# Expert 0's first steps placed behind each reading of the stop, ahead of the jump out of the tiles

## The reference

```
X = np.fft.fft(np.fft.fft(x, axis=1), axis=2).real       # x: 4 x 3072 x 256
...
k = np.maximum(xk @ w_k, 0.0); v = k * k @ w_v            # xk, xr: mixes with the row before
r = 1.0 / (1.0 + np.exp(-(xr @ w_r)))
x = (r * v).reshape(B * S, 256)                           # 12288 rows
...
expert_idx = np.argmax(x @ w_gate, axis=1)                # 8 experts
for i in range(N):
    e = expert_idx[i]
    if counts[e] < capacity:                              # capacity = 384
        disp[e, counts[e]] = x[i]
        ...
h = np.maximum(np.einsum('ecd,edf->ecf', disp, w1), 0.0)
y = np.einsum('ecf,efd->ecd', h, w2)
out[i] = gate_w[i] * y[expert_idx[i], pos[i]]             # 0 for rows that were not kept
```

## Time and profile before

| what | us |
|---|---|
| median of 3 runs | 610.83 |
| lowest and highest | 610.41, 610.84 |
| the profiled execution's own time | 610.44 |
| its span in the profile | 608.6 |
| PE busy | 597.7 (98% of the span) |
| DVE busy | 449.9 (74%) |
| ACT busy | 317.1 (52%) |
| POOL busy | 103.5 (17%) |

### The profile page before, as it was taken

One profiled execution on the slowest core, in us unless ns is written; L12 is line 12 of the kernel. 1 busy time (PEld: TensorE's weight loads), 2 busy tenths in 40 slices (PEclk: granted clock), 3 DMA queues, 4 the chain that ended last, 5 costly groups with the idle time before them and its releaser, 6 DMA issues.

```text
span 608.6 us, 10524 instructions
## 1 busy us (share of the span) xinstructions
PE 597.7 (98%) x3368; PEld 515.6 (85%) x3368; DVE 449.9 (74%) x1054; ACT 317.1 (52%) x668; POOL 103.5 (17%) x105
## 2 busy tenths in 40 slices
PE   8999999999999999999999999999999999999995
PEld 5878888888888788888888888788888999999995
DVE  4688888887777688889786767788884777766671
ACT  1774645454545564545454545564544565665550
POOL 0710302020202020202020202020207111011111
PEclk9999999999999999999999999999999999999999
DMA  8439946241510005201010100033105944455000
GB/s 309 151 86 186 394 147 205 93 139 53 184 52 23 2 10 195 94 1 43 23 37 2 34 1 3 29 118 122 30 1 174 326 129 140 144 191 189 28 26 26
DMA packets 42157, 62.99 MB, mean 103 GB/s; under 512 B 4582, under 2 KB 32055, under 8 KB 42108
## 3 DMA queue, kind: packets, MB, share of 16 engines
q1 hardware_dynamic: 38268, 55.88, 29.0%
q0 software_dynamic: 3840, 6.52, 3.0%
HBM read 39.90 MB, written 26.91 MB: 110 GB/s over the span
## 4 chain that ended last, share of the span: by engine, by line
PE 94%; DVE 1%; SPq 1%; issue 1%; DMA 1%; ACT 1%; POOL 0%; POOLq 0%; DVEq 0%; ACTq 0%
PE bank L299 77%; PE bank L1305 4%; PE bank L1252 3%; PE bank L1264 2%; PE bank L1237 2%; DMA first_partner<-in_x 1%; PE bank L1499 1%; PE bank L1337 1%; PE bank L1508 1%; DVE xt L928 0%; PE bank L1512 0%; PE bank L1509 0%; SPq L475 0%; SPq L486 0%; PE bank L1350 0%
## 5 line engine op out<-in xcount | busy, mean ns | idle before, releaser
L299 PE MATMUL bank<-k,wv 128*128 128x512 f32 x672 | 165.3, 396 | 0.0
L299 PE MATMUL bank<-xk,wk 128*128 128x512 f32 x642 | 164.1, 399 | 0.0
L299 PEld LDWEIGHTS bank<-k,wv 128*128 128x128 f32 x672 | 125.6, 188 | 28.9
L299 PEld LDWEIGHTS bank<-xk,wk 128*128 128x128 f32 x642 | 118.7, 189 | 25.7
L761 ACT ACTIVATE relu<-bank 128x512 f32<-128x512 f32 x114 | 67.9, 597 | 118.7 <-PE bank L299 110.1
L629 POOL DMA_INDIRECT dispatched<-rows,slot x56 | 59.2, 1057 | 371.2 <-DVE slot L1028 324.0
L1047 DVE TENSOR_TENSOR square<-relu 128x512 f32<-128x512 f32 x113 | 78.0, 691 | 32.9 <-ACT relu L761 23.7
L1042 DVE TENSOR_TENSOR k<-square,k 128x512 fp32r<-128x512 f32 x112 | 76.7, 685 | 2.9 <-ACT k L756 2.7
L756 ACT ACTIVATE k<-square 128x512 fp32r<-128x512 f32 x113 | 70.7, 626 | 10.7 <-DVE square L1047 10.2
L299 PE MATMUL bank<-down_w,he 128*128 128x256 f32 x576 | 71.9, 284 | 0.0
L299 PEld LDWEIGHTS bank<-down_w,he 128*128 128x128 f32 x576 | 70.4, 191 | 0.0
(11 more groups left out here) (142 smaller groups left out, 721.3 us busy)
## 6 DMA issues: line engine op xcount, KB each, us to landing
out_rows<-blank SPq DMA_DIRECT2D x16, 768.0 KB
raw_up<-in_moe_w SPq DMA_DIRECT2D x8, 1024.0 KB, 22.4
raw_down<-in_moe_w SPq DMA_DIRECT2D x8, 1024.0 KB
got<-dispatched SPq DMA_DIRECT2D x16, 409.5 KB, 3.2
x_area<-in_x SPq DMA_DIRECT2D x12, 384.0 KB
y<-in_x SPq DMA_DIRECT2D x9, 384.0 KB
dispatched<-blank SPq DMA_DIRECT2D x1, 3276.0 KB, 21.4
first_partner<-in_x SPq DMA_DIRECT2D x3, 384.0 KB
```

Of the source, the lines that this page charges most:

```text
L299: done = nc.tensor.matmul(bank, w, x, start=first and i == 0, stop=last and i == len(terms) - 1)
```

## The change

`walk` gets a fifth function, `leave`. Behind the reading of the stop, the case "full" now comes first: it holds `leave()` and then a jump to behind the tiles. The case "not full" stands behind that jump (`Else`), so an engine that goes on takes a branch over `leave`.

```
-    def walk(eng, before, after, last):
+    def walk(eng, before, after, last, leave):
...
                 eng.load(stop, full[0:1, n + 1:n + 2])
-                with eng.If_eq(stop, 0):
+                with eng.If_ne(stop, 0):
+                    leave()
+                with eng.Else():
                     rest(n)
...
                 last()
+                leave()
...
-                walk(sp, before, after, last)
-
-                sp.sem_inc(rows_in[0], 16)
+                walk(sp, before, after, last, lambda: sp.sem_inc(rows_in[0], 16))
...
-                walk(pool, before, lambda n: None, lambda: route(NTILE - 1))
+                walk(pool, before, lambda n: None, lambda: route(NTILE - 1), lambda: pool.sem_inc(waits_held, 1))
...
-                walk(act, before, after, lambda: route(NTILE - 1))
-                nc.scalar.activation(warm[:, 2:3], warm[:, 1:2], ACT.Copy).then_inc(act_left, 1)
+                def turned(e, i):
+                    for h in range(DH):
+                        act.wait_ge(te_full, e * DH + h + 1)
+                        nc.scalar.activation(xe[:, i, 0, h, :], tbe[h][:, 0:cap], ACT.Copy).then_inc(xe_high, 1)
+
+                def leave():
+                    nc.scalar.activation(warm[:, 2:3], warm[:, 1:2], ACT.Copy).then_inc(act_left, 1)
+                    turned(0, 0)
+                    nc.scalar.activation(warm[:, 0:1], warm[:, 1:2], ACT.Exp)
+
+                walk(act, before, after, lambda: route(NTILE - 1), leave)
...
-                turned(0, 0)
                 act.wait_ge(dve_left, 1)
...
-                walk(dve, before, after, last)
-                nc.vector.memset(least[:, :], 0.0).then_inc(dve_left, 1)
...
+                def leave():
+                    nc.vector.memset(least[:, :], 0.0).then_inc(dve_left, 1)
+                    turned(0, 0)
+
+                walk(dve, before, after, last, leave)
 
                 dve.sem_inc(he_ready, 3)
                 dve.sem_inc(ye_ready, SP)
...
                 dve.sem_inc(we_ready, PIECES)
-                turned(0, 0)
                 dve.wait_ge(act_left, 1)
...
                         up(n, 2)
                         up(n, 3)
+
+                def after(n):
+                    seq, stage = n // TILES + 1, stage_of(n)
                     if n % TILES:
                         up(n, 2)
-
-                def after(n):
-                    seq, stage = n // TILES + 1, stage_of(n)
...
-                walk(pe, before, after, last)
-
...
+                def leave():
+                    turn(0, 0, 0)
+                    pe.wait_ge(act_left, 1)
+                    keep_warm_with(5, ident, ident, hbe[1])
+
+                walk(pe, before, after, last, leave)
...
-                turn(0, 0, 0)
-                pe.wait_ge(act_left, 1)
-                keep_warm_with(3, ident, ident, hbe[1])
-                pe.wait_ge(dve_left, 1)
                 with pe.Fori(0, EXPERTS // 2) as turn_no:
```

More of the change, by code:

```diff
@@ L1164, in last, with turned @@
                     dve.wait_ge(routed, NTILE + 2)
-                walk(dve, before, after, last)
-                nc.vector.memset(least[:, :], 0.0).then_inc(dve_left, 1)
+                def turned(e, i):
+                    for h in range(DH):
+                        dve.wait_ge(xe_high, e * DH + h + 1)
+                        nc.vector.tensor_tensor(xe[:, i, 1, h, :], tbe[h][:, 0:cap], xe[:, i, 0, h, :].bitcast(fp32), ALU.subtract).then_inc(xe_ready, 1)
+                def leave():
+                    nc.vector.memset(least[:, :], 0.0).then_inc(dve_left, 1)
+                    turned(0, 0)
+                walk(dve, before, after, last, leave)
                 dve.sem_inc(he_ready, 3)
@@ L1176, in weights @@
                         nc.vector.tensor_tensor(low, raw, high.bitcast(fp32), ALU.subtract).then_inc(we_ready, 1)
[L1178 to L1182, removed]
                 def gates(e, i):
```

## The result

The changed kernel takes **616.29 us** (median of 6 runs, 615.46 to 616.82) against 610.84 before (6 runs, 610.41 to 611.31): ratio **1.0089, 95% interval 1.0076 to 1.0102**. It is slower by 5.4 us, where +1.0 was forecast and the range ended at +3.1. The profiled execution took 616.13 us, with a span of 614.3 us (before 610.44 and 608.6): 5.7 us to explain.

The account below looks back on a forecast made before the run. PE was taken as the bound, through when expert 0's first product begins: 0.9 us later start, 0.1 back in that product, 0.2 for the fetch under load, so +1.0 on the 610.83 median: 611.8 us, range 610.4 to 613.9.

Parts of the forecast that it names:

- What bounds the kernel, and where the change acts: PE, busy 597.7 of 608.6 us; only the start of expert 0's first product, at 461.73, was said to matter.
- Everything behind it shifts with it: On PE, all work after expert 0's first product was to move by the same delay as its start.
- DVE's jump comes at 459.1: Leaving the tiles, DVE's jump waits for ACT's second copy and starts at 459.1, not 458.1: 1.0 us later.
- run past its waits: Rival: DVE's sequencer jumps at about 458.3 without waiting for its subtractions; no change, -0.2, 610.6 us, chance 0.10.
- The same 3.1 us, so 462.2 and the first product at 462.6: DVE's jump keeps its length, DVE resumes at 462.2, and expert 0's first product begins 0.9 us later than 461.73.
- PE and ACT aren't last: PE resumes between 460.1 and 462.1, ACT's jump ends at 461.6, both ahead of DVE's 462.2.
- `up(14, 2)` gone, branches over `leave` at nothing: Dropping PE's 1.56 us of vain work gains nothing; 0.25 us more per branch in tiles 6 to 13 costs nothing.
- The fetch under the weights' load: Expert 1's weights, asked for 3.0 us sooner, flow during DVE's jump fetch: 0 to 2.2 us, taken as 0.2.
- the upper bound of 2.2: Most that DVE's jump fetch could lose: a load of `got` lands in 5.3 us beside the weights, normally 3.2.
- The clock: Rival: PE's 3.0 us gap before the first product lowers its clock, about 2.1 us; +2.9, 613.7 us, chance 0.06.
- the late fetch: Rival: DVE's jump fetch waits behind the queued 2 MB of weights, up to 2.2 us; +3.0, 613.8 us, chance 0.20.

Follow-up runs that it names:

- weights late and PE busy: Changed kernel, but SP asks for expert 1's weights once DVE is behind its jump, and 7 idle products follow PE's jump: 611.27 us, ratio 1.0015.
- the run with `raw_up` alone: Changed kernel with 16 more idle products behind PE's jump and only the first weight load (1 MB) asked for early: one execution, 614.67 or 614.80 us.
- PE busy, +4.5: Changed kernel with 16 more idle products behind PE's jump, weights asked for as early as in the change: 614.86 us, ratio 1.0073.
- the signals alone: Changed kernel with DVE's signals raised ahead of its jump and two wider idle products for five, weights still asked for early: 611.77 us, ratio 1.0027.

## Why the prediction was wrong

Point by point, by its own steps:

- **What bounds the kernel, and where the change acts:** right for 3.33 of the 5.7 us, by which the first product begins later. "Everything behind it shifts with it" was not: another 2.38 us arise behind that start, at half clock.
- **DVE's jump comes at 459.1:** right to 0.1 us. The second copy ended at 459.07, the jump began at 459.1. DVE didn't run past its waits, so that rival is out.
- **The same 3.1 us, so 462.2 and the first product at 462.6:** right where the weights had not been asked for ahead of the jump (462.0 and 462.50 with weights late and PE busy), wrong in the change itself (464.6 and 465.06).
- **PE and ACT aren't last:** right. PE's jump ended at 460.7 (460.1 to 462.1 forecast); ACT's next signals came at 461.5 (461.6 forecast).
- **`up(14, 2)` gone, branches over `leave` at nothing:** right. PE's branches in the tiles took 0.20 to 0.34 us between 250 and 450 us, in place of 0.06, but the gate's products end only 0.05 us later than before, and between 220 and 450 us PE is busy for 229.76 of 230 us (before 229.75).
- **The fetch under the weights' load, "I take 0.2, nearer to zero, because the fetch comes ahead of the full stream":** this is the step that failed. It measured **2.4 us** (5.5 against 3.1), beyond the upper bound of 2.2 (its two rows, 5.3 and 3.2, give 2.1). The request for the weights went out 0.7 us ahead of the jump, and that decides: with the request 0.2, 0.7 or 1.0 us behind the jump's start, the jump took 3.0 to 3.3 us. I read the wrong column of the earlier trace rows: 262 GB/s come 1.9 us behind the issue, but the DMA share is 1.31 already 0.9 us behind it. In the change the share is 0.82 in the jump's first microsecond, while 82 GB/s move. That a fetch is held up by how busy the engines are, and not by how much lands, is my reading; it isn't the whole cause, since in the run with `raw_up` alone the delay outlasts the busy engines by 2.4 us.
- **The clock:** its price was about right (2.1 forecast, 2.38 measured at half clock in the profiled execution), its chance and its place were not, and this is the second step that failed. I took the fall for an alternative to the late fetch, at 0.06. But every microsecond by which DVE is late makes PE's gap longer: 3.0 us in my own sum, 5.45 in the end. The two rivals are one chain, 0.9 + 2.4 + 2.4 = 5.7 us, and no case of mine held both, so the range ended at 613.9. My own upper prices together would have given 0.8 + 2.2 + 2.1 = 5.1 us, 615.9. "No stretch that I read has a granted clock below 1.00" was no evidence: it was read from a kernel whose gap is 0.95 us.

On the fetch behind the weights the Trainium skill says (DMA: Bandwidth & Descriptors, "Queues, rings and completion order"): a DMA engine serves its queues in turn, a whole packet at a time. The longer jumps (5.5 us against 3.1) when the weights are in line first agree with it; that half the bytes cost as much, and that DVE resumed 2.4 us after the weights had landed, it does not explain.

And the Trainium skill's warning that a long idle gap between bursts of matmuls brings the lower clock back (TensorE: Matmul & The Clock Gate, "Why this matters for your kernels") agrees with the change's gap of 5.45 us, behind which the granted clock stands at 0.50. Gaps of 2.1 to 2.9 us cost the clock here too, in some executions.

What each part is worth in the medians against before: the jump behind the subtractions +0.9 (weights late, PE busy); the weights ahead of the jump +3.6 more (PE busy, +4.5), of which 2.6 are the jump (5.5 against 2.9) and 0.45 PE's wait behind it, while the remaining 0.5 us is in no trace, as the profiled execution was the fastest of its kernel (613.96); the clock +1.0 on top (the change, +5.4). At half clock PE doesn't meet DVE's loop, so the last two overlap. The idea of the change, the chain of transposes, copies and low parts ahead of the jump, pays here only with the other half: what PE waits for is signalled ahead of the jump too, and the loads are asked for behind its start. Either half alone was slower than before (611.77 with the signals alone, 611.27 with the loads and idle products alone). That version gains 0.7 us (609.70 against 610.41) where the change loses 5.4.

## What to carry to other kernels

A far jump waits for transfers of instructions that go through the DMA engines: look at what was asked of these in the microsecond before it, and ask for big loads behind it. Look at the next step that fetches as well, since a load asked for behind the jump can stand ahead of that one (2.2 us against 5.1 at DVE's loop). Raise every signal that doesn't depend on the code behind a jump ahead of the jump. And when two slower cases feed each other (a late signal, a longer gap on PE, a lower clock), add their prices for the upper end of the range instead of choosing between them.

## What the runs showed of the hardware

- **A far jump** took 2.9 to 3.3 us on DVE when the weights had not been asked for ahead of it (seven kernels, the one before among them), and 5.5 to 6.5 us when 1 or 2 MB had been asked for some 0.7 us ahead (five kernels). PE's took 3.3 to 3.9; in all twelve it started at least 1.2 us ahead of the request for the weights.
- **The same loop can have a fetch at its start or not.** In the change and in six edits DVE's step into its loop took 1.8 to 3.0 us, in one of them 5.1 (under load); in the kernel before and in four edits with slightly other code ahead of the loop 0.2. The instructions of the loop are the same, only their place in the program differs. That a block's edge falls there is my reading; no run moved it on purpose.
- **The clock:** no profiled execution shows it fall at gaps on PE up to 1.6 us. Two profiles show a fall, with gaps of 2.14 and 5.45 us. By times and mean clocks it fell in 4 of 11 executions with a gap of 2.1 us, in 2 of 11 with 2.4, 3 of 4 with 2.6, 4 of 5 with 2.9, and in all 6 with 5.45.
